# One reordered hand-over: the second half of the first attention step moves ahead of the feed-forward work, with two products in the accumulator banks

## The reference, cut to what matters

```python
# delta-rule attention: 4 x 8 heads, 768 tokens, head dimension 48
for t in range(S):
    y[:, :, t] = q_t @ state                       # read before the update
    v_old = state^T k_t
    state = state + beta_t * outer(k_t, v_t - v_old)
# then two feed-forward networks over 3072 tokens x 384 features
h = x @ w_in                                       # 384 -> 2048
g = where(h >= 1, h, where(h <= -1, 0, (h + 1)**2 / 4))
x = g @ w_out                                      # 2048 -> 384
xn = x / rms(x) * rms_g                            # 384 -> 1536, gate and value
y = (silu(xn @ w_gate) * (xn @ w_val)) @ w_out2
```

## Time and profile before

| | |
|---|---|
| median of three runs | 1073.98 us |
| profiled execution | 1073.82 us |
| its span | 1072.0 us |
| TensorE busy | 1041.4 us (97%) |
| VectorE busy | 580.2 us (54%) |
| ScalarE busy | 427.9 us (40%) |
| granted TensorE clock | 0.998 of 2.4 GHz |

### The profile page before, as it was taken

The page is one execution under the profiler, slowest core; times in us unless marked ns, Lnnn a source line. Parts: engine busy times, 40 slices in busy tenths (PEclk is TensorE's granted clock), DMA queues, the critical chain, the costliest instruction groups (busy, mean ns, idle before and its releaser), DMA issues.

```text
span 1072.0 us, 24895 instructions
## 1 busy us (share of the span) xinstructions
PE 1041.4 (97%) x11116; PEld 861.0 (80%) x11116; DVE 580.2 (54%) x1017; ACT 427.9 (40%) x728; POOL 9.6 (1%) x20
## 2 busy tenths in 40 slices
PE   6999999999999999999999999999999999999996
PEld 3589888777777777777778888888888888888885
DVE  5978769858947848863356435324324234333322
ACT  5745534443454454353476543132232232232211
POOL 1000000000000000000000000000000000000000
PEclk9999999999999999999999999999999999999999
DMA  8604004102300410030030230200200200100101
GB/s 245 173 4 118 3 4 124 26 4 61 89 3 3 119 31 3 31 120 2 2 119 30 89 118 1 59 1 1 60 1 2 59 1 1 30 1 1 30 1 29
DMA packets 19033, 48.08 MB, mean 45 GB/s; under 512 B 2448, under 2 KB 9232, under 8 KB 17872
## 3 DMA queue, kind: packets, MB, share of 16 engines
q1 hardware_dynamic: 18928, 46.51, 15.7%
HBM read 37.06 MB, written 9.44 MB: 43 GB/s over the span
## 4 chain that ended last, share of the span: by engine, by line
PE 80%; DVE 12%; issue 3%; ACT 2%; DMA 2%; SPq 0%; DVEq 0%; ACTq 0%
PE bank L690 21%; PE hps L1235 14%; PE acc L1250 13%; PE acc L709 10%; PE hps L690 7%; PE hps L709 4%; DVE outer L992 3%; DVE inv L996 2%; DVE g L1065 2%; PE acc L1268 2%; DVE g1l L1073 2%; PE bank L1194 1%; PE bank L1180 1%; PE bank L1173 1%; DVE tt L1006 1%
## 5 line engine op out<-in xcount | busy, mean ns | idle before, releaser
L607 ACT ACTIVATE g<-bank 128x512 f32<-128x512 f32 x72 | 43.1, 599 | 257.2 <-PE bank L690 142.6
L1235 PE MATMUL hps<-xh,w1h 128*128 128x512 f32 (+1 forms) x336 | 129.9, 387 | 4.0 <-DVE g L1065 3.0
L895 ACT ACTIVATE g1h<-g 128x512 fp32r<-128x512 f32 (+1 forms) x112 | 63.9, 571 | 169.4 <-DVE g L1065 144.6
L1250 PE MATMUL acc<-g1h,w2h 128*128 128x512 f32 (+1 forms) x336 | 127.7, 380 | 1.7 <-DVE g1l L1073 1.4
L1235 PE MATMUL hps<-xh,w1l 128*128 128x512 f32 (+1 forms) x336 | 122.0, 363 | 0.0
L1250 PE MATMUL acc<-g1h,w2l 128*128 128x512 f32 (+1 forms) x336 | 122.0, 363 | 0.0
L1235 PE MATMUL hps<-xl,w1h 128*128 128x512 f32 (+1 forms) x336 | 121.9, 363 | 0.0
L1250 PE MATMUL acc<-g1l,w2h 128*128 128x512 f32 (+1 forms) x336 | 121.8, 363 | 0.0
L1073 DVE TENSOR_TENSOR g1l<-g,g1h 128x512 fp32r<-128x512 f32 (+1 forms) x112 | 68.6, 613 | 71.0 <-ACT g1h L895 70.4
L1065 DVE SCALAR_TENSOR_TENSOR g<-hps,g 128x512 f32<-128x512 f32 (+1 forms) x112 | 68.1, 608 | 50.9 <-ACT g L889 50.5
L886 ACT ACTIVATE g<-hps,half_c 128x512 f32<-128x512 f32 (+1 forms) x112 | 69.7, 622 | 55.7 <-PE hps L1235 55.6
(11 more groups left out here) (173 smaller groups left out, 2044.4 us busy)
## 6 DMA issues: line engine op xcount, KB each, us to landing
kqT<-kq SPq DMA_DIRECT2D x22, 384.0 KB, 6.4
v_in<-v SPq DMA_DIRECT2D x6, 768.0 KB, 4.6
k_in<-k SPq DMA_DIRECT2D x6, 768.0 KB, 5.5
x2d<-x2s SPq DMA_DIRECT2D x18, 256.0 KB, 5.5
x2t<-x2d SPq DMA_DIRECT2D x6, 768.0 KB, 5.9
y<-y_t SPq DMA_DIRECT2D x48, 96.0 KB, 2.2
stage<-w_in SPq DMA_DIRECT2D x4, 768.0 KB, 8.3
stage<-w_out SPq DMA_DIRECT2D x4, 768.0 KB, 8.7
```

Source lines behind the costliest of these rows:

```text
L607: act.activation(silu[:, f % 2, :], gps[f % 2][:, :], ACT.Silu).then_inc(e_silu, 1)
L895: act.activation(g1h[:, f % 2, 0:WIDTH[n]], g1[:, f % 2, 0:WIDTH[n]], ACT.Copy).then_inc(s_gh, 1)
L1235: last = pe.matmul(hps[f % 2][:, 0:WIDTH[n]], wt[:, kk, P * f:P * f + P], xx[:, kk, COLS[n]], start=(kk == 0 and e == 0), stop=(kk == KD - ...
L1250: last = pe.matmul(acc[j][:, 0:WIDTH[n]], wt[:, f, P * j:P * j + P], gg[:, f % 2, 0:WIDTH[n]], start=(f == 0 and e == 0), stop=(f == NF1 - ...
```

## The change

Four things are altered, all in the lists of order:

- In `first_body()` the last two weight pieces, 22 and 23, stand side by side behind the two `X` products. `GQ` of the second half (written GQ(0,1): step 0, half 1) and `KU` of the first half (KU(0,0)) come into this body from the one behind it.
- `FIRST` places them: GQ(0,1) in `acc1` and `acc2`, KU(0,0) in `acc0` and bank 0. Other banks shift in consequence.
- Because `acc0` to `acc2` now hold them, the first unit that writes an accumulator, `o0` of tile 0 and block 0, waits for two more counts: `s_state` (KU(0,0) evicted) and `s_gq` at `NQ` = 4 (all four parts of the two `GQ` evicted).
- `second_half()` moves its other events ahead by one to three units, and `GQE` of the second half from unit 8 to unit 13. `LEAD` is 480 and no longer 530, so that the inversion of step 1 ends at unit 127 where it ended at unit 115.

```diff
@@ first_body
-    out += [("ft", 0, 0), ("Z", 0, 0), ("Z", 0, 1), ("piece", 0, NPIECE - 2), ("xd", 0, 0), ("X", 0, 0), ("X", 0, 1)]
-    out += [("ft", 0, 1), ("ft", 0, 2), ("vnh", 0, 0), ("low", 0, NPIECE - 2), ("GQE", 0, 0), ("U", 0, 0), ("piece", 0, NPIECE - 1)]
-    out += [("trh", 1, 0), ("PU", 0, 0), ("low", 0, NPIECE - 1)] + [("XT", 0, n) for n in range(KD)] + [("XE", 0, n) for n in range(KD)]
+    out += [("ft", 0, 0), ("Z", 0, 0), ("Z", 0, 1), ("xd", 0, 0), ("X", 0, 0), ("X", 0, 1), ("ft", 0, 1), ("ft", 0, 2), ("vnh", 0, 0)]
+    out += [("piece", 0, NPIECE - 2), ("piece", 0, NPIECE - 1), ("low", 0, NPIECE - 2), ("GQE", 0, 0), ("U", 0, 0), ("low", 0, NPIECE - 1), ("GQ", 0, 1), ("trh", 1, 0)]
+    out += [("PU", 0, 0), ("KU", 0, 0)] + [("XT", 0, n) for n in range(KD)] + [("XE", 0, n) for n in range(KD)]
@@ second_half
-    return [(1, ("KU", 0, 0)), (2, ("vnh", 0, 1)), (5, ("KS", 0, 1)), (8, ("GQ", 0, 1)), (8, ("GQE", 0, 1)), (13, ("U", 0, 1)),
-            (16, ("QS", 0, 1)), (21, ("PU", 0, 1)), (24, ("KU", 0, 1))] + ...
-LEAD = 530
+    return [(0, ("vnh", 0, 1)), (4, ("KS", 0, 1)), (11, ("U", 0, 1)), (13, ("QS", 0, 1)), (13, ("GQE", 0, 1)), (18, ("PU", 0, 1)),
+            (21, ("KU", 0, 1))] + ...
+LEAD = 480
@@ FIRST
-         ("PU", 0, 0): (1, 2), ("XT", 0, 0): (3,), ("XT", 0, 1): (4,), ("XT", 0, 2): (0,), ("KU", 0, 0): (1, 2)}
+         ("GQ", 0, 1): (6, 7), ("PU", 0, 0): (1, 2), ("KU", 0, 0): (5, 0), ("XT", 0, 0): (3,), ("XT", 0, 1): (4,),
+         ("XT", 0, 2): (1,), ("KS", 0, 1): (2, 0)}
@@ forward, on TensorE
                             if j == 0 and n == 0 and f == 0:
                                 pe.wait_ge(s_wl, PIECES * NCHUNK)
+                                pe.wait_ge(s_state, MEM)
+                                pe.wait_ge(s_gq, NQ)
```

More of the change, by code:

```diff
@@ L133, in first_body @@
     out += split(2) + [("low", 0, NPIECE - 4), ("low", 0, NPIECE - 3)]
-    out += [("ft", 0, 0), ("Z", 0, 0), ("Z", 0, 1), ("piece", 0, NPIECE - 2), ("xd", 0, 0), ("X", 0, 0), ("X", 0, 1)]
-    out += [("ft", 0, 1), ("ft", 0, 2), ("vnh", 0, 0), ("low", 0, NPIECE - 2), ("GQE", 0, 0), ("U", 0, 0), ("piece", 0, NPIECE - 1)]
-    out += [("trh", 1, 0), ("PU", 0, 0), ("low", 0, NPIECE - 1)] + [("XT", 0, n) for n in range(KD)] + [("XE", 0, n) for n in range(KD)]
+    out += [("ft", 0, 0), ("Z", 0, 0), ("Z", 0, 1), ("xd", 0, 0), ("X", 0, 0), ("X", 0, 1), ("ft", 0, 1), ("ft", 0, 2), ("vnh", 0, 0)]
+    out += [("piece", 0, NPIECE - 2), ("piece", 0, NPIECE - 1), ("low", 0, NPIECE - 2), ("GQE", 0, 0), ("U", 0, 0), ("low", 0, NPIECE - 1), ("GQ", 0, 1), ("trh", 1, 0)]
+    out += [("PU", 0, 0), ("KU", 0, 0)] + [("XT", 0, n) for n in range(KD)] + [("XE", 0, n) for n in range(KD)]
     return out, [(("trh", 1, n), 10) for n in range(1, 6)] + [e for e in inversion(1)[:-1] if e[0][0] != "tr" and e[0] not in (("ft", 1, 1), ("ft", 1, 2))] +         inversion(1)[-1:] + [(("ft", 1, n), 20) for n in range(1, TURNS)]
 def second_half():
-    return [(1, ("KU", 0, 0)), (2, ("vnh", 0, 1)), (5, ("KS", 0, 1)), (8, ("GQ", 0, 1)), (8, ("GQE", 0, 1)), (13, ("U", 0, 1)),
-            (16, ("QS", 0, 1)), (21, ("PU", 0, 1)), (24, ("KU", 0, 1))] +         [(33 + n, ("XT", 1, n)) for n in range(KD)] + [(35, ("XE", 1, n)) for n in range(KD)]
-LEAD = 530
+    return [(0, ("vnh", 0, 1)), (4, ("KS", 0, 1)), (11, ("U", 0, 1)), (13, ("QS", 0, 1)), (13, ("GQE", 0, 1)), (18, ("PU", 0, 1)),
+            (21, ("KU", 0, 1))] + [(32 + n, ("XT", 1, n)) for n in range(KD)] + [(34, ("XE", 1, n)) for n in range(KD)]
+LEAD = 480
 DENSE = 570
```

## The result

The changed kernel takes 1086.89 us (median of 4 runs, 1085.67 to 1087.35) where the kernel before took 1074.76 in the same series: ratio 1.0111, 95% interval [1.0094, 1.0129]. It is 12.1 us slower; 3.45 were forecast.

What follows compares the result with a forecast made beforehand. TensorE, busy nearly throughout, was taken as the bound, with VectorE the source of stalls. Stall net of hand-over +3.95, inversion -0.9, serial chain +0.1, later steps +0.3: +3.45 on 1073.82, predicted 1077.2 us, range 1073.9 to 1080.2.

Steps and rivals of the forecast that it cites:

- the direction: Whole kernel: the change makes it slower, given 63%, against 30% for no change and 7% for faster.
- the stall at the first `o0`: TensorE waits there for GQE(0,1), behind the third clip on VectorE's list: 4.5 us, or 3.95 net of the hand-over's gain.
- The wait of 1.2 us for `w2l`: Hand-over: GQ(0,1) waits until piece 23 is stored by ScalarE, so TensorE does nothing for 1.2 us.
- the inversion: Wider inversion, units 38 to 127: fewer waits for VectorE, partly offset by two wide transposes, -0.9 us.
- Up to here the change gains 0.5: Hand-over up to `h0`: `h0` 2.0 us late, but with GQ(0,1) and KU(0,0) done, worth 2.5 us.
- Rival 2: Behind the stall at the first `o0` TensorE comes back at 1.2 GHz: 2.5 us more, 1079.7 us; chance 18%.
- the serial chain of step 1: Its 18 products have 35 units beside them instead of 48; waits that go and waits that grow sum to +0.1 us.
- the later steps: Four pairs of the next inversion move from tile 1 to tile 2: +0.3 us.
- `gram`: Serial chain of step 1: the wait of 1.40 us for it, from two transposes in a row on VectorE, should go.
- KS's wait: Serial chain of step 1: it grows from 1.11 to about 2.0 us, behind a clip; the second KS waits 0.3 more.
- Rivals 1 and 3: First `o0`: 1 (24%), VectorE gives the stall back, 1074.8 us; 3 (8%), counts met in time, no stall, 1070.7 us.
- the forecast's 50: Chance of 50% given to the main forecast, own range 1075.8 to 1078.6 us; 45 counted as slower, 4 as no change.

Runs made afterwards that it cites:

- e1: Changed kernel with GQE(0,1) moved from unit 13 to right behind the XE parts of the first tile: 1080.35 us, ratio 1.0074.
- e5: Kernel before with GQE(0,1) moved to unit 13 and the first `o0` waiting for it, the stall alone: 1080.59 us, ratio 1.0052.
- e11: Changed kernel with its first unit of 64 small products, GK(0,0), issued twice in idle time at the start: 1087.44 us, ratio 1.0117.
- e4: Kernel before with only weight pieces 22 and 23 moved, behind the two `X` and ahead of U(0,0): 1078.83 us, ratio 1.0034.
- e6: Kernel before with only KU(0,0) moved, from behind the first `h0` to right behind PU(0,0): 1074.63 us, ratio 1.0001.
- e3: Changed kernel with `LEAD` back at 530: 1085.32 us, ratio 1.0091.
- e8: Kernel before with the first `o0` waiting for GQE(0,1), which stays at unit 8, so a shorter stall: 1077.79 us, ratio 1.0029.
- e2: Kernel before with `LEAD` 480 instead of 530 and nothing else: 1078.06 us, ratio 1.0024.
- e9: Kernel before with `LEAD` 580 instead of 530: 1071.93 us, ratio 0.9973.
- e7: Changed kernel with GQE(0,1) right behind the hand-over, piece 22 back between `Z` and `X`, and `LEAD` 530: 1076.63 us, ratio 1.0016.
- e10: The kernel of e7 with KU(0,0) also back at unit 1, behind the first `h0`: 1076.42 us, ratio 1.0011.
- e12: Kernel before with `LEAD` 640 instead of 530: 1073.58 us, ratio 0.9978.

## Why the prediction was right and wrong

**Right: the direction, and the stall at the first `o0`.** Its working gave 4.5 us and the trace has 4.45, with VectorE's list in the order and at the durations that were read from rows of before. That VectorE's list decides when TensorE goes on was the step with most weight, and e1 and e5 confirm it by taking it away and by adding it alone. The wait of 1.2 us for `w2l` was right, and so was the inversion: -0.9 forecast, -1.2 measured, with waits of 1.3 us.

**Wrong: "Up to here the change gains 0.5".** The hand-over cost 2.0 at equal products. The step took the duration of each product and each wait for another engine, and left out TensorE's own supply of instructions. The two "issue" waits are 2.68 us, and e11, which has neither, is 2.8 us shorter in this stretch. e4 and e6 show that each rearranged row brings one by itself, and e1, e3 and e4 that the clock can fall there too, which adds some 2 to 3 us. The trace of before had such waits in sight, of 0.2 to 0.7 us, in rows of small products, and the prediction did not read them.

**Wrong: Rival 2's mechanism was taken for the less likely case.** The stall did cost clock: 0.50 behind it, +1.8 us at equal products to the next `XT` (+2.05 in e5), against the 2.5 that the rival worked out. The argument against it, that the idle time at the start doesn't show that a pause takes the clock away, was true of that trace and no reason to expect that it would not. (The full clock that the views list ahead of 19.4 us, and that this rival mentions, is no reading: the trace's record of the clock begins there.) The Trainium skill (TensorE: Matmul & The Clock Gate, "HAM oscillation — how this bites in real kernels") says that a TensorE left without work for long enough falls back to half rate; the runs agree for the stalls of 3.22 and 4.45 us; behind 1.46 us in e8 it did not fall back, behind 1.59 us in e4 it did.

**Wrong in size: the serial chain of step 1 (+0.1, measured +2.5) and the later steps (+0.3, measured +1.2).** The forecast gave `gram` as gone and KS's wait as grown. `gram` went; KS's wait is 1.76 us in e2, near the 2.0 forecast, and 0.26 in the changed kernel. What the step left out is that the same rows of 64 small products, with 13 units less between them, run into "issue" waits: 1.7 us of them and two falls of the clock in the changed kernel, 2.2 us of them and no fall in e2, against 1.1 us before. e2 has the same +2.4 and so shows that it is all `LEAD`, and e9 that the opposite direction gives 2.0 us. How the +2.4 divides among these is not shown, nor what the +1.2 of the later steps is made of. In the step on the wider inversion the remark that `Z` used to give VectorE time between the two wide transposes is a slip: `Z` stood behind both then too, at unit 132.

**Rivals 1 and 3** fell. VectorE gave back 0.5 us behind the stall of 1.46 (e8), and nothing that shows behind the two longer ones, where the lower clock may hide it. The counts were not met in time.

Row by row of the table, the misses are +0.2 (start), +2.5 (hand-over), +0.1 (stall), +1.8, -0.3, +2.4, +0.9 and -0.1: 7.5 us, which with the forecast 3.45 make the profiled execution's 11.0. (In the chances of the prediction the forecast's 50 is shared out as 45 and 4; one point is missing.)

**Open.** Why the clock falls behind some short waits and not behind others, and what sets off the long stretch at the lower clock in some executions of e1; and why the packet of instructions that e11 waits for (last section) set out so late. No experiment here tells that.

## What to carry to other kernels

A wait placed on TensorE costs its length and, when the clock falls with it, some 2 us more at half clock (each of the five waits of 3.2 to 4.5 us in mid-run did that here, and some of the shorter ones); read from the list of the engine that releases it how long it will be, and move that engine's work first. Rows of small products are cheap only with wide ones between them: packed together they run into waits for instructions that no other engine's work shows, so spread pieces and units among them rather than gather them (e7 and e10, where that took the waits away one by one, took 1076.6 and 1076.4 us, still no less than before). When a planner's constant is changed, try it in the other direction as well; here that was the only part that paid.

## What the runs showed of the hardware

**Waits for instructions stand on a grid of 256.** Counted in recorded matmuls in order of start, "issue" waits stood at 343 to 345 (seven kernels), 467 (e9, e10), 594 (after, e1, e3, e4), 846 (after, e1, e3, e6, e7), 973 (e11) and 1098 (before), whatever work stands there. Each matmul has one weight load (11116 of each on the page of the changed kernel). Counted with the loads and TensorE's few sequencer instructions, these places are 707, 962, 1218, 1731, 1986 and 2242: 255 or 256 apart, and 513 where one between them brought no wait. Of all 57 "issue" waits in the first 180 us of the fourteen profiles 46 stand on this grid; the others are one of 0.68 to 0.69 us at matmul 2558 in eight kernels and three of about 0.3 us, and what those are is not known. The page names the packets that bring the instructions:

```profile
q8 instruction: 87, 1.43, 0.5%
```

In the trace each of them has 16384 bytes, and each of the 46 waits ends 1.2 to 1.7 us after one of them has landed. The size of a wait is then how much earlier TensorE came to the place: in the changed kernel the packet for place 343 landed at 37.9 us and TensorE went on at 39.4 after 0.17 us; in e11 TensorE stood at the same place from 32.5 us, the packet landed at 35.7, and TensorE went on at 37.0. From one place of the grid to going on at the next took 3.2 to 3.7 us in the long waits of the hand-over, while two rows of 64 products (128 instructions and 1.08 us each) come to the next place in some 2.2. That leaves 1.0 to 1.5 us of waiting by this estimate, and 0.95 to 1.59 were measured; a piece of 1.28 us between the rows hides most of it.

The Trainium skill (Runtime: NRT & Kernel Launch, "Instruction fetch mechanics") says that an engine's instructions are brought in blocks of 256, and that crossing into the next is mostly hidden. The spacing agrees. "Mostly hidden" holds beside wide products, and in rows of small ones these runs show 0.2 to 1.6 us, once 4.51.

**The clock falls behind standing still, and not only behind long stalls.** In the profiled executions all five waits of 3.2 to 4.5 us from 30 us on (after, e3, e5, and two in e11) came with 3.4 to 10 us at 0.50. Of those of 2.1 to 2.8 us four did (e1, e5, e8, e12) and two did not (e2, e7); of those of 1.1 to 1.7 us three did (1.32 in e1, 1.59 in e3 and e4) and the rest did not, 1.46 in e8 among them. It also fell in stretches where TensorE was listed as busy for 2.4 to 2.7 of 3 us with small products, and for 24 us in one execution of e1 with TensorE listed as busy for 23.75 of them; in e9 it fell at 48.8 us, a microsecond behind a wait of 0.53. Runs of one kernel differ accordingly: e2 took 1075.5 us with a mean clock of 0.998 and 1082.7 with 0.986.
